# Attention and two feed-forward layers in one kernel: V products of two steps in one run, reciprocals spread by a transpose, unrolled batches, a reordered prologue

## The reference

```python
B, H, S, D = 4, 8, 576, 64          # attention, causal, with a decay bias
scores = q @ k.T / sqrt(D) + min(-(cum[i] - cum[j]), 0), causal mask
attn = exp(scores - max) / (sum + 1e-9)
x = (attn @ v), laid out as (B*S, H*D) = (2304, 512)
xn = x / sqrt(mean(x*x) + 1e-6) * rms_g
x = (silu(xn @ w_gate) * (xn @ w_val)) @ w_out        # d_ff 1536
out = (h - tanh(h)) @ w2_out, h = x @ w2_in           # d_ff 2048
```

## Time and profile before

| | |
|---|---|
| median of 3 runs | 1106.84 us (1105.74 to 1106.98) |
| profiled execution: time | 1111.58 us |
| profiled execution: span of the trace | 1109.8 us |
| PE busy | 1080.0 us, 97% |
| DVE busy | 444.0 us, 40% |
| ACT busy | 418.7 us, 38% |
| POOL busy | 168.4 us, 15% |
| PE's last product of attention ends at | 248.5 us |
| granted PE clock, mean | 0.99 |

### The profile page before, as it was taken

The page is one execution under the profiler, slowest core; times in us unless marked ns, Lnnn a source line. Parts: engine busy times, 40 slices in busy tenths (PEclk is TensorE's granted clock), DMA queues, the critical chain, the costliest instruction groups (busy, mean ns, idle before and its releaser), DMA issues.

```text
span 1109.8 us, 19419 instructions
## 1 busy us (share of the span) xinstructions
PE 1080.0 (97%) x6836; PEld 998.6 (90%) x6836; DVE 444.0 (40%) x1214; ACT 418.7 (38%) x1030; POOL 168.4 (15%) x178
## 2 busy tenths in 40 slices
PE   4999999899999999999999999999999999999998
PEld 3888787789999999999999999999999999899997
DVE  6677677554432321321322333433223232332322
ACT  4676667664422232222222233433223232332322
POOL 4777777730000000000000000000000000000000
PEclk9999999899999999999999999999999999999999
DMA  5444455213200000000000122310000000000000
GB/s 187 150 150 150 154 157 152 85 32 96 67 1 1 1 0 0 0 0 0 0 0 0 29 76 77 95 29 29 1 1 29 0 28 0 0 28 0 28 0 28
DMA packets 48452, 51.66 MB, mean 47 GB/s; under 512 B 2990, under 2 KB 38830, under 8 KB 48394
## 3 DMA queue, kind: packets, MB, share of 16 engines
q1 hardware_dynamic: 48394, 50.94, 14.8%
HBM read 41.63 MB, written 4.87 MB: 42 GB/s over the span
## 4 chain that ended last, share of the span: by engine, by line
PE 95%; issue 1%; DVE 1%; DMA 1%; POOL 1%; ACT 1%; SPq 0%; ACTq 0%; DVEq 0%; POOLq 0%
PE HP L954 15%; PE HP L956 15%; PE HP L955 15%; PE YP L955 11%; PE YP L956 11%; PE YP L954 11%; PE TP L892 5%; PE OP L908 5%; PE SC L879 4%; PE OP L920 2%; PE SC L880 2%; DMA Qraw<-in_qT 0%; ACT PT L451 0%; DMA QO<-QA 0%; PE MP L927 0%
## 5 line engine op out<-in xcount | busy, mean ns | idle before, releaser
L954 PE MATMUL HP<-XS,WA 128*128 128x384 f32 x576 | 194.6, 338 | 0.3 <-ACT AC L518 0.3
L956 PE MATMUL HP<-XS,WA 128*128 128x384 f32 x576 | 193.0, 335 | 0.0
L955 PE MATMUL HP<-XS,WA 128*128 128x384 f32 x576 | 192.7, 335 | 0.0
L760 DVE TENSOR_TENSOR AC<-AC,HP 128x384 f32<-128x384 f32 (+2 forms) x78 | 40.3, 523 | 294.1 <-PE HP L956 294.1
L811 DVE TENSOR_TENSOR AC<-HP,AC 128x384 f32<-128x384 f32 (+1 forms) x108 | 54.3, 512 | 216.3 <-ACT AC L580 216.3
L580 ACT ACTIVATE AC<-HP 128x384 f32<-128x384 f32 x96 | 47.2, 492 | 215.7 <-PE HP L956 215.2
L954 PEld LDWEIGHTS HP<-XS,WA 128*128 128x128 f32 x576 | 108.2, 188 | 3.0 <-issue 0.5
L955 PEld LDWEIGHTS HP<-XS,WA 128*128 128x128 f32 x576 | 108.2, 188 | 2.4
L956 PEld LDWEIGHTS HP<-XS,WA 128*128 128x128 f32 x576 | 108.1, 188 | 0.0
L518 ACT ACTIVATE AC<-HP 128x384 f32<-128x384 f32 x72 | 35.4, 492 | 178.3 <-PE HP L956 178.3
L954 PE MATMUL YP<-HS,WX 128*128 128x384 f32 (+2 forms) x312 | 102.1, 327 | 0.5 <-DVE HS L766 0.5
(11 more groups left out here) (109 smaller groups left out, 2029.3 us busy)
## 6 DMA issues: line engine op xcount, KB each, us to landing
X<-in_w SPq DMA_DIRECT2D x52, 256.0 KB, 3.3
Kraw<-in_kT SPq DMA_DIRECT2D x16, 576.0 KB, 4.8
Qraw<-in_qT SPq DMA_DIRECT2D x16, 576.0 KB, 5.6
out_rows<-OS SPq DMA_DIRECT2D x18, 256.0 KB, 2.2
QO<-QA SPq DMA_DIRECT2D x15, 288.0 KB, 3.3
Vt<-in_v SPq DMA_DIRECT2D x16, 256.0 KB, 3.1
WRAW<-in_w SPq DMA_DIRECT2D x16, 256.0 KB, 2.8
Vt<-in_v SPq DMA_DIRECT2D x16, 32.0 KB, 2.1
```

The lines of the kernel that those rows point to most:

```text
L760: dve.tensor_tensor(AC[:, m % 2, cols], AC[:, m % 2, cols], HP[:, 1, cols], ALU.mult).then_inc(prod_done if part is None else prod_part, 1)
L954: pe.matmul(dst, w(0), x(0), start=start, stop=False)
L955: pe.matmul(dst, w(0), x(1), start=False, stop=False)
L956: return pe.matmul(dst, w(1), x(0), start=False, stop=stop)
```

## The change

What it does:

- `values` for two steps are issued together in every odd step, `spread` for two steps together in every even one. `output` and `spread_out` follow in pairs. `PT` has 3 buffers now and `PR` 3.
- `spread` is one transpose of 128 columns (`RW`, into both heads' partitions at once) in place of two products. `RW` is `RR` copied 64 times for each head by DVE, right behind the reciprocal.
- The batches are written out on all engines; there is no loop in attention.
- POOL's low parts no longer wait for `qo_in`.
- The loads of pair 1 are issued ahead of the waits for `cum_hi` and `cum_lo`; four memsets of `QO` and `Vt` and two of `onesm` and `eps` go from DVE to POOL, and the memsets of `PR` go behind the cumulated sums.

```diff
-        PR = sb("PR", [P, 4, 2, PAD + S], F32)
-        PT = sb("PT", [P, 2, 2, QB * P], F32)
+        PR = sb("PR", [P, 3, 2, PAD + S], F32)
+        PT = sb("PT", [P, 3, 2, QB * P], F32)
+        RW = sb("RW", [P, 4, 2, D], F32)
...
             load_qk(0, 0, 0)
+            load_qk(0, 1, 1)
             for row, part in enumerate((cum_hi, cum_lo)):
...
-            load_qk(0, 1, 1)
...
-                pool.wait_ge(qo_in[j], 16 * (2 * b + p // 2 + j))
                 pool.wait_ge(k_hi, 2 * k)
...
                 dve.reciprocal(RR[0:z, n % 4], RE[0:z, n % 4]).then_inc(recip_done, 1)
+                dve.wait_ge(recip_done, b * STEPS + n + 1)
+                wait(dve, spread_mm, b * STEPS + n - 3)
+                dve.nop(nofuse=True)
+                dve.tensor_copy(RW[0:z, n % 4], RR[0:z, n % 4].rearrange("p (h o) -> p h o", o=1)
+                                .broadcast_to([z, 2, D])).then_inc(wide_done, 1)
...
-                    if n > V_LAG or not first:
-                        output(b, n - V_LAG - 1)
+                    if n % 2 == 0:
+                        for m in (n - V_LAG - 2, n - V_LAG - 1):
+                            if m >= 0 or not first:
+                                output(b, m)
...
-                pe.wait_ge(recip_done, b * STEPS + n + 1)
+                pe.wait_ge(wide_done, b * STEPS + n + 1)
                 wait(pe, o_evac, b * STEPS + n - 1)
                 pe.nop(nofuse=True)
-                for hh in range(2):
-                    last = pe.matmul(OP[hh * D:(hh + 1) * D, n % 2, 0:z],
-                                     RR[:, n % 4, hh:hh + 1].broadcast_to([P, D]), ident[:, 0:z],
-                                     start=True, stop=True)
-                last.then_inc(spread_mm, 1)
+                pe.transpose(OP[:, n % 2, 0:z],
+                             RW[0:z, n % 4].rearrange("p h d -> p (h d)"), ident[0:z, 0:z]).then_inc(spread_mm, 1)
...
-                    if n >= R_LAG or not first:
-                        spread(b, n - R_LAG)
-                    if n >= V_LAG or not first:
-                        values(b, n - V_LAG)
-
-            batch(0, first=True)
-            with pe.Fori(1, B - 1) as b:
-                batch(b)
-            batch(B - 1, last=True)
+                    if n % 2 == 0:
+                        for m in (n - R_LAG - 1, n - R_LAG):
+                            if m >= 0 or not first:
+                                spread(b, m)
+                    else:
+                        for m in (n - V_LAG - 1, n - V_LAG):
+                            if m >= 0 or not first:
+                                values(b, m)
+
+            for b in range(B):
+                batch(b, first=(b == 0), last=(b == B - 1))
```

More of the change, by code:

```diff
@@ L293, in _ @@
             sp.wait_ge(cum_out, 32)
[L295 to L299, removed]
+            for k in range(B * PAIRS):
+                at, after = divmod(k + 1, PAIRS), divmod(k + 2, PAIRS)
+                if k + 1 < B * PAIRS:
+                    wait(sp, scores_done, 2 * QB * k)
                     load_decay(*at)
-                    sp.wait_ge(q_hi, 2 * (b * PAIRS + p + 2))
+                    sp.wait_ge(q_hi, 2 * (k + 2))
                     load_qo(*at)
-                if not last or p + 2 < PAIRS:
-                    if isinstance(b, int) and b * PAIRS + p == 0:
+                if k + 2 < B * PAIRS:
+                    if k == 0:
                         sp.wait_ge(qo_first, 2)
@@ L308, in load_ahead @@
                     else:
[L309 to L316, removed]
-                    load_weights(*after)
[L319 to L325, removed]
+                        sp.wait_ge(k_lo, 2 * k)
+                        sp.wait_ge(q_lo, 2 * k)
+                    load_qk(*after, k % 2)
+                if k + 1 < B * PAIRS:
+                    wait(sp, pv_done, QB * k)
+                    load_v(*at, (k + 1) % 2)
+                if k + 2 < B * PAIRS:
+                    sp.wait_ge(w_lo, k + 1)
+                    load_weights(*after)
             for k, (src, _, i, sem_free, count) in enumerate(loads):
@@ L358, in _ @@
                                base=0, pattern=[[-1, P]], channel_multiplier=1).then_inc(consts, 1)
+            pool.wait_ge(consts, 2)
+            for j in range(2):
+                pool.memset(QO[D:D + 2, j].bitcast(F32), 1.0).then_inc(padded, 1)
+            for j in range(2):
+                pool.wait_ge(padded, j + 2)
+                pool.memset(Vt[0:P - PAD, j, 0, :], 0.0).then_inc(padded, 1)
+            pool.wait_ge(padded, 4)
             def prepare(b, p):
@@ L405, in _ @@
                 pool.tensor_scalar(QA[:, 0, hh], Qraw[:, 0, hh], 1.0, 1.0, ALU.mult, ALU.mult).then_inc(q_hi, 1)
[L406 to L409 removed]
+            pool.memset(onesm[:], 1.0 / DM).then_inc(onesm_set, 1)
+            pool.memset(eps[:], RMS_EPS).then_inc(onesm_set, 1)
+            for b in range(B):
+                batch(b, last=(b == B - 1))
             pool.wait_ge(gcol_in, 16)
@@ L502, in _ @@
                 act.activation(QO[0:D, 0, hh], Qraw[0:D, 0, hh], ACT.Copy).then_inc(qo_first, 1)
-            batch(0, first=True)
[L504 to L509, removed]
-                    for hh in range(2):
-                        evacuate(B, n - T_LAG, hh)
+            for b in range(B):
+                batch(b, first=(b == 0), last=(b == B - 1))
+            for hh in range(2):
+                evacuate(B, -2, hh)
+            spread_out(B, -3)
+            spread_out(B, -2)
+            for hh in range(2):
+                evacuate(B, -1, hh)
+            spread_out(B, -1)
             def silu(c, m):
@@ L642, in _ @@
                                      ).then_inc(cum_step, 1)
-            dve.memset(onesm[:], 1.0 / DM).then_inc(onesm_set, 1)
-            dve.memset(eps[:], RMS_EPS).then_inc(onesm_set, 1)
+            for j in range(3):
+                dve.memset(PR[:, j, :, 0:PAD], 0.0).then_inc(pr_padded, 1)
             def minima(b, n, hh):
@@ L743, in _ @@
             dve.wait_ge(eps_set, 1)
[L744 to L747, removed]
+            for b in range(B):
+                batch(b, first=(b == 0), last=(b == B - 1))
             recip(B, -1)
[L749 to L753, removed]
+            for n in (-5, -4):
+                output(B, n)
+            for hh in range(2):
+                evacuate(B, -2, hh)
+            for n in (-3, -2):
+                output(B, n)
+            for hh in range(2):
+                evacuate(B, -1, hh)
+            output(B, -1)
             def product(c, m):
```

52 lines of the change are left out of this document (24 added, 28 removed).

## The result

The changed kernel takes 1149.42 us in the median (1148.83 to 1151.15, 4 runs), the kernel before 1106.43 us beside it (1105.74 to 1106.98, 4 runs): a ratio of 1.039, 95% interval 1.038 to 1.040. It is 43.0 us slower, where +28 us and 1135 us were forecast; 1149 lies in the range.

The account below looks back on a forecast made before the run. PE was taken to set the pace, but not alone, with DVE and POOL close behind. Gains of -11 and +39 us from held-up DVE copies made +28: 1139.6 us against the profiled execution, 1135 for the median, range 1092 to 1152.

Parts of the forecast that it names:

- The main step: DVE's copy RW<-RR stands still while a POOL instruction runs: 0.20 plus 0.45 us a copy, 3.3 us a pair.
- The pace: Attention pairs 1 to 13: 15.4 us plus 0.8 of lost clock, 3.0 more than before, +39 us in all.
- A visit to the other shape: PE's change to the 64-column shape and back: 0.34 us each; 40 visits in place of 80, -13.6 us.
- the way in: Part of a visit: PE's change to the 64-column shape, 0.15 us.
- the way back: Part of a visit: the first scores product after V comes 0.33 us later in place of 0.14, making 0.19.
- the spread as a transpose: One transpose on PE in place of the spread products: -7.9 us, against +7.0 for 64-row transposes as a third shape.
- -11.0 us: Gains beside the steady pairs: -1.2 prologue start, -6.7 POOL's wait and clock in pair 1, -3.1 loop's turn.
- the last two pairs: End of attention, where ACT and the end of POOL's work set the pace: left as they are.
- Not held up: Rival: POOL doesn't hold up DVE's copy; pairs stay near 13.1 us, 1095 us; chance 0.26.
- PE alone: Rival: DVE has room and PE alone sets the pace, 12.3 us a pair, 1081 us; chance 0.05.
- swallowed: Rival: copies held up, but fewer meet POOL and DVE's waits are used; 1104 to 1112, at most 1119; chance 0.13.
- The clock stays down: Rival: half of all pairs' time granted 1.2 GHz, PE's 12.3 us over 18, above 1160 us; chance 0.04.

Follow-up runs that it names:

- by another form: The changed kernel with a DVE tensor reduce over one element writing RW in place of the copy: 1108.53 us, ratio 1.002.
- by less POOL: The changed kernel with POOL's high and low parts cut to 72 of 576 columns from the third pair on: 1110.46 us, ratio 1.0035.
- ACT's copy: The changed kernel with the copy into RW made by ACT, between the step's two exponentials, in place of DVE: 1095.8 us, ratio 0.990.
- the unpaired kernel: The changed kernel with RW written by ACT, and V products, spreads, RB copies and outputs one step at a time: 1095.28 us, ratio 0.990.
- the two runs: The kernel before, with only the prologue reordered and POOL's QO wait removed: 1102.14 us; with only the batch loops written out: 1104.89 us.
- the reduction in the kernel before: The kernel before plus a DVE tensor reduce writing RW behind each reciprocal, 80 times, with no reader: 1122.1 us, ratio 1.015.

## Why the forecast was right, and where it was off

**The main step holds.** The forecast was +28 us, the measured change +43.0. Copies of 0.23 us beside idle POOL and up to 1.47 beside its instructions; 0.648 us in the mean, where 0.65 were worked out from rows of other operations. The pace was to be 15.4 plus 0.8 of clock; pairs 2 to 11 take 16.27 in the mean, 3.1 more than a steady pair of before, for 3.0 forecast. Hold-up and place were each taken away alone, the length only together with the hold-up:

- length and hold-up both off DVE: -53.6 us
- only the hold-up gone, by another form: -40.9; by less POOL: -39.0
- only the place changed, the hold-up left: -43.3

These don't add up, as each removes the same thing: a long instruction ahead of a `PT` copy. A hold-up costs most where PE soon waits behind it: held up but last in the step, the copies do no worse (1106.1 us) than the reductions that are never held up in the old place (1108.5). And DVE's length alone has a price there: 12.7 us between the reduction and ACT's copy (of two groups; 14.2 by their ratios), some 0.16 us for each write of 0.29.

**The gains were mis-sized on PE.** "A visit to the other shape costs 0.34 us" is wrong: 0.08 by the waits above, nothing in the time. Of its two parts the 0.19 us for "the way back" is paid after transposes as well, so fewer visits don't save it; of the 0.15 for the way in, starts show 0.09 or 0.18, by what they are compared with. I had read ends, which are modelled, and compared with the second product in place of a first one. So the -13.6 us weren't there, and the spread as a transpose, net -0.9 by my sum, is worth more: 0.45 us a pair, about 7 us (12.9 without waits before, 12.45 in the unpaired kernel). The two errors cancel: 12.25 us for PE alone stands beside my 12.3, and that is luck. In the median the spread with ACT's copy shows as some 5.5 us (1100.8 by the kernel before less the terms of the batches and the prologue, if these add up, to 1095.3).

**Prologue, POOL, loop.** Of -11.0 us the two runs show -4.1 (interval of the ratio: -2.9 to -6.4) and -1.4 (-4.0 to +0.6), half of it. In the traces the loop's turn and the second pair are saved as forecast, the start is not: the first product at 10.89 in place of 11.36 is 0.5 us, not 1.2, since the four `KD` transfers end last as before. The trace that I worked from exaggerates: the profiled execution of before was 4.7 us over its median, that of the changed kernel 0.6 under. I took what its pairs lost as if each execution lost it. Two later traces bear on that. At the loop's turn the 3.1 us were 1.5 of waiting and 1.6 of clock; in the run with the new prologue, which keeps the loop, the pair there costs 2.1 us and loses no clock. And one of the last pairs, number 14, was this in the trace of before:

```profile
204.63:224.34 19.71, 17.23 (x136) 13.87 (x135) 11.01 (x45) 12.28 (x33) 13.22 (x15) 0.74 0.17 45
```

With the batches written out and with the new prologue the same pair takes 15.57 and 15.55 us at a clock of 1.00. These 4 us of lost clock are near the 4.7 of the offset; that the other executions of before are without them is not shown, as they have no trace.

**The 14.4 us by which the forecast fell short.** The profiled times differ by 37.3 us where 28.0 were forecast, 9.2 more; the other 5.2 are that offset (4.7 carried over and 0.6 found, less rounding). Pair by pair the surplus is: first product +0.7, pair 0 +0.6, pair 1 -1.8, pairs 2 to 12 +0.9, pair 13 +1.1, the last two +7.9, and -0.2 behind attention. So the term that was mis-sized is "the last two pairs, where ACT and the end of POOL's work set the pace, I leave as they are": it was put at nothing. They take 22.56 and 29.3 us where the trace of before has 19.71 and 24.2. The copy stands in them as in the others, and the mean clock is 0.62 in the first of them. With ACT's copy they take 17.5 and 25.0, with DVE's copy last in the step 17.8 and 26.0, so most of the surplus comes from the copy in its place; against the 15.6 us of pair 14 at the full clock it would be 4 us larger. Which wait ends last there the trace doesn't name ("issue", up to 1.80 us). The longest of these ends at 238.16, when a `PT` copy of ACT, behind a table load of 1.28 us, and one of DVE, behind a held-up copy of 1.40, end within 0.3 us of each other; their shares stay open.

**The rivals.** *Not held up*, 1095 us: its premise is refuted, yet 1096 is what comes when the write leaves DVE. Its other part, that an unheld copy costs nearly nothing, fails too: the reduction, only 0.07 us longer than a free copy, gives 1108.5. *PE alone*, 1081, and *swallowed*, up to 1119, didn't come; 1106 is what the copy at the step's end gives, beside held-up copies. *The clock stays down*: from the first product to the last of attention the mean granted clock is 0.90, which makes a fifth of the time at the lower level, not half. (Its price was off too: half of the time at the lower level would make 16.4 us of 12.3, not over 18.)

## What to carry to other kernels

Before an instruction is given to an engine "with room", ask what stands behind it in that engine's queue and who waits for it: the same 80 copies, held up alike, make a kernel of 1149.4 us ahead of a copy PE needs and one of 1106.1 behind it. They are not free there either: written by ACT they leave 1095.8. A VectorE copy from SBUF to SBUF beside GpSimd work is priced by GpSimd's instruction (0.22 to 1.47 us here), not by its size; ScalarE did it in 0.29 to 0.32 each time. The price of a visit to another tile shape is to be taken from a run with fewer visits: a gap in a timeline can be the length of the instructions themselves.

## Not expected of the hardware

- A tensor reduction over one element takes 0.277 to 0.289 us for 128 elements, POOL busy or not, where the plain copy takes 0.22 to 1.47.
- Where the loop goes round, one more DVE instruction a step made the turn far dearer. The pair there took 22.81 us with the reduction in the kernel before, 13.87 its neighbour: 8.9 us, where before it was 3.1 (and 22.20 with the copy, 7.0 to 7.3 over its neighbours). With the reduction DVE had a second gap with no releaser, 5.7 us after the first (its timeline in that kernel):

```profile
127.56 0.29 DVE L700 TENSOR_TENSOR X<-OP,RB 128x128 f32 x1 [2.22 <-issue]
...
133.23 0.36 DVE L662 CUSTOM_DVE_ANT_0 PR<-SC,mask 128x192 f32<-128x192 f32 x1 [3.38 <-issue]
```

- PE's clock fell to 1.2 GHz after one wait of 1.71 us; with waits of 0.38 and 0.51 us at the same step, the copy standing last, the V products that follow ran at the full rate (28 records in 1.75 us, where the changed kernel took 3.26).
